# Fifteen block products instead of eighteen: the first layers from expert 1 on by a Hopcroft-Kerr scheme, in a three-stage kernel on one Trainium2 core

## The reference

```python
def _attn_ref(r, k, v, w, u):                      # (2, 8, 768, 48)
    for t in range(S):
        cur = einsum('bhd,bhe->bhde', u * k_t, v_t)
        y[:, :, t] = einsum('bhd,bhde->bhe', r_t, state + cur)
        state = w * state + einsum('bhd,bhe->bhde', k_t, v_t)

def _moe_ref(x, domain_probs, w1, w2):             # x (1536, 384), w1 (4, 384, 1024)
    p = domain_probs / (domain_probs.sum(-1, keepdims=True) + 1e-09)
    for e in range(E):
        out += p[:, e:e + 1] * (np.maximum(x @ w1[e], 0.0) @ w2[e])

def _moe2_ref(x, w_in, w_out):                     # w_in (384, 2048), w_out (2048, 384)
    h = x @ w_in
    return (h * (1.0 / (1.0 + np.exp(-1.702 * h)))) @ w_out
```

## Time and profile before

| what | value |
|---|---|
| median of 3 runs | 642.78 us (642.29 to 642.92) |
| span of the profiled execution, first to last instruction | 640.5 us |
| PE busy | 635.2 us, 3880 matmuls |
| VectorE busy | 222.4 us |
| ScalarE busy | 203.4 us |
| GpSimd busy | 170.0 us |
| granted TensorE clock, mean | 1.000 |

### The profile page before, as it was taken

How to read it: one execution, slowest core, us unless ns; L and a number is a source line. 1 busy time by engine, 2 the same in 40 slices (tenths; PEclk the granted TensorE clock), 3 DMA queues, 4 the chain that set the end, 5 groups by cost and what they waited for, 6 DMA issues and landing times.

```text
span 640.5 us, 9440 instructions
## 1 busy us (share of the span) xinstructions
PE 635.2 (99%) x3880; PEld 529.3 (83%) x3880; DVE 222.4 (35%) x369; ACT 203.4 (32%) x421; POOL 170.0 (27%) x168
## 2 busy tenths in 40 slices
PE   8999999999999999999999999999999999999998
PEld 6999888888888888888888888888888888888886
DVE  8987642212121212121212121213533333333332
ACT  4744432332222212222211223223643333333223
POOL 5664300342242303242402245422750000000000
PEclk9999999999999999999999999999999999999999
DMA  8765521006000501000310000220000010001001
GB/s 331 278 217 189 202 115 51 4 1 247 1 0 1 196 2 49 2 0 1 151 47 1 0 1 0 98 101 1 2 0 1 3 47 1 0 2 50 1 0 50
DMA packets 8722, 39.08 MB, mean 61 GB/s; under 512 B 1504, under 2 KB 1632, under 8 KB 7392
## 3 DMA queue, kind: packets, MB, share of 16 engines
q1 hardware_dynamic: 8672, 38.40, 15.9%
HBM read 36.01 MB, written 2.38 MB: 60 GB/s over the span
## 4 chain that ended last, share of the span: by engine, by line
PE 98%; DVE 1%; DMA 0%; issue 0%; ACT 0%; DVEq 0%
PE bank L1097 46%; PE bank L1123 31%; PE bank L1139 15%; PE bank L1171 2%; PE bank L1215 1%; PE bank L1218 1%; PE bank L1205 1%; PE bank L1190 1%; PE bank L1208 0%; DMA wu_sb<-wu_rows 0%; DVE w_pow L800 0%; DVE q_k_mid L816 0%; PE bank L1223 0%; DVE q_tab_k L807 0%; DVE acc L951 0%
## 5 line engine op out<-in xcount | busy, mean ns | idle before, releaser
L1097 PE MATMUL bank<-x_hi,w_hi 128*128 128x512 f32 (+1 forms) x456 | 172.5, 378 | 0.0
L1097 PE MATMUL bank<-x_lo,w_hi 128*128 128x512 f32 (+1 forms) x456 | 172.4, 378 | 0.0
L1097 PE MATMUL bank<-x_hi,w_lo 128*128 128x512 f32 (+1 forms) x456 | 172.3, 378 | 0.0
L876 DVE SCALAR_TENSOR_TENSOR h_lo<-bank,h_hi 128x512 fp32r<-128x512 f32 (+1 forms) x104 | 67.5, 649 | 257.3 <-ACT h_hi L700 257.3
L700 ACT ACTIVATE h_hi<-bank 128x512 fp32r<-128x512 f32 (+1 forms) x104 | 58.7, 564 | 286.6 <-PE bank L1097 286.6
L622 POOL TENSOR_TENSOR w_lo<-staging,w_hi 128x384 fp32r<-128x384 f32 x80 | 82.2, 1039 | 173.4 <-ACT w_hi L670 173.4
L1123 PE MATMUL bank<-h_hi,w_hi 128*128 128x512 f32 (+1 forms) x312 | 117.7, 377 | 0.1
L1123 PE MATMUL bank<-h_hi,w_lo 128*128 128x512 f32 (+1 forms) x312 | 116.3, 373 | 0.0
L1123 PE MATMUL bank<-h_lo,w_hi 128*128 128x512 f32 (+1 forms) x312 | 116.3, 373 | 0.0
L1097 PEld LDWEIGHTS bank<-x_hi,w_hi 128*128 128x128 f32 x456 | 85.8, 188 | 15.9
L1097 PEld LDWEIGHTS bank<-x_hi,w_lo 128*128 128x128 f32 x456 | 85.8, 188 | 15.8
(11 more groups left out here) (86 smaller groups left out, 433.4 us busy)
## 6 DMA issues: line engine op xcount, KB each, us to landing
staging<-weights SPq DMA_DIRECT2D x10, 1536.0 KB, 8.7
rkv_in<-rkv_n SPq DMA_DIRECT2D x10, 640.0 KB, 5.5
rk_in<-rk_t SPq DMA_DIRECT2D x12, 512.0 KB, 5.2
staging<-weights SPq DMA_DIRECT2D x4, 768.0 KB, 8.9
p_bc<-p_normalised SPq DMA_DIRECT2D x4, 768.0 KB, 4.2
out<-p_bc SPq DMA_DIRECT2D x9, 256.0 KB, 2.1
rkv_in<-rkv_n SPq DMA_DIRECT2D x2, 448.0 KB, 5.7
u_bc<-u_rows SPq DMA_DIRECT2D x1, 192.0 KB, 11.7
```

The costliest lines, as they stand in the source:

```text
L876: dve.scalar_tensor_tensor(h_lo[:, slot, 0:size], hid, 0.0, h_hi[:, slot, 0:size].bitcast(F32), ALU.max, ALU.subtract).then_inc(sem["hlo"], 1)
L1097: last = pe.matmul(bank[:, HID[j % 2], 0:tokens.stop - tokens.start], w[:, k, :], xs[c][:, k, tokens], start=(n == 0), stop=(n == 3 * KT - 1))
```

## The change

Experts 1 to 3 and the second feed-forward block are worked in **pairs** of hidden tiles: a pair q is two hidden tiles by all three token blocks, four pairs to a stage, 20 in all (0 to 11 the experts, 12 to 19 the second block). The first layer of a pair is a product of a 2 x 3 matrix of weight blocks by a 3 x 3 matrix of x blocks (128 features by 512 tokens). Written plainly that is 18 block products of three matmuls. The new kernel uses 15: each multiplies a sum of weight blocks (12 sums, made anew per pair, `weight_sums`) or a weight block itself by a sum of x blocks (8 summed blocks, made once for the experts by `form(0, ...)` and once for the second feed-forward block by `form(1, ...)`, rounded and split by `sum_high` and `sums_low`) or an x block.

A product writes one of three banks (5, 6, 7; the third column of `PRODUCT`). Where `begins` is False it adds to what is there. Behind each product the bank is read once: by ScalarE, which copies it, with a sign, to one of eight result buffers t (`take`, 6 per pair), or by VectorE, which adds or subtracts it (`join`, 9 per pair). When the last product of a result is in, ScalarE rounds it (`high`) and VectorE, in the second block GpSimd, makes the low part (`low`). In the second block sigmoid (`silu`, ScalarE) and `gate` (VectorE) come before.

The second layer of a pair is nine **groups** of 6 matmuls (token block n, output tile k; two hidden tiles by three passes). For n = 0 they stay in PSUM over the four pairs of a stage, for n = 1 and 2 they leave after every pair (`leave` on VectorE, the exit; for the experts then `gather` on GpSimd). In the list of the program five products of pair q + 1 follow one group of pair q, then come two groups more and the next, and so on. Pair 12 (`PLAIN`), the first of the second feed-forward block, has its first layer done plainly, in 6 products of 9 matmuls, since its input is only then finished; it comes between the groups of pair 11 (which all leave), and pair 13 is mixed into it in another pattern. Weights are loaded per pair (384 KB for each layer) in place of per stage. The sums of blocks for the second block stand in VectorE's queue behind the third gate of pair 12, their low parts in GpSimd's at the same place of the list.

```diff
-STEPS1 = MOE_BLOCKS * FT
-STEPS = STEPS1 + BLOCKS * F2 // P
+STEPS = len(SPANS) * FT
...
+ONE, LONG, SHORT = 7, 5, 6
+PRODUCT = (
+    (0, (1, 1), ONE, True, "copy", 1, 1),
+    (1, 13, LONG, True, "copy", 4, -1),
+    (2, (0, 0), SHORT, True, "copy", 0, 1),
+    (3, (2, 1), LONG, False, "add", 1, -1),
+    (12, 8, SHORT, False, "add", 1, -1),
+    (4, (1, 0), ONE, True, "add", 0, 1),
+    (13, 14, LONG, False, "add", 0, 1),
+    (5, 3, SHORT, False, "copy", 2, 1),
+    (6, 9, LONG, False, "copy", 3, 1),
+    (7, (2, 2), ONE, True, "copy", 5, -1),
+    (8, (0, 2), SHORT, False, "add", 5, 1),
+    (9, 1, ONE, False, "add", 3, -1),
+    (14, 10, LONG, False, "add", 5, 1),
+    (10, 4, SHORT, False, "add", 4, -1),
+    (11, (1, 2), LONG, False, "add", 2, 1),
+)
+SUM_HOME = {13: 0, 8: 1, 14: 2, 3: 3, 9: 4, 1: 5, 10: (0, 1), 4: (2, 0)}
+SUM_ORDER = (13, 8, 14, 3, 9, 1, 10, 4)
...
+def pairs():
+    order = [("product", 0, i) for i in range(PRODUCTS)]
+    begin = {0: 0}
+    def mix(q, lead):
+        begin[q + 1] = len(order)
+        left = iter(range(PRODUCTS))
+        for n, takes in enumerate(lead):
+            if n:
+                order.append(("group", q, *divmod(n - 1, KT)))
+            order.extend(("product", q + 1, next(left)) for _ in range(takes))
+    for q in range(PLAIN - 1):
+        mix(q, (0, 5, 0, 0, 5, 0, 0, 5, 0, 0))
+    q = PLAIN - 1
+    begin[PLAIN] = len(order)
+    order += [("group", q, n, k) for n in range(2) for k in range(KT)] + [("plain", PLAIN, i) for i in range(2)]
+    order += [("group", q, 2, k) for k in range(KT)] + [("plain", PLAIN, i) for i in range(2, 6)]
+    mix(PLAIN, (0, 0, 0, 0, 0, 2, 1, 2, 2, 8))
+    for q in range(PLAIN + 1, ALL_PAIRS - 1):
+        mix(q, (0, 5, 0, 0, 5, 0, 0, 5, 0, 0))
+    begin[ALL_PAIRS] = len(order)
+    order += [("group", ALL_PAIRS - 1, n, k) for n in range(BLOCKS) for k in range(KT)]
+    after = [[] for _ in range(len(order) + 8)]
+    for at, (what, q, *rest) in enumerate(order):
+        if what == "product" and rest[0] in (LAST_OF[o] for o in DONE):
+            pos = DONE.index(PRODUCT[rest[0]][5])
+        elif what == "plain":
+            pos = rest[0]
+        else:
+            if what == "group" and q == PLAIN - 1:
+                after[at + 2].append(("rest", q, *rest))
+            continue
+        later = iter(range(at + 1, at + 5))
+        if q >= MOE_PAIRS:
+            after[next(later)].append(("silu", q, pos))
+            after[next(later)].append(("gate", q, pos))
+        after[next(later)].append(("high", q, pos))
+        after[next(later)].append(("low", q, pos))
+    for q in range(1, ALL_PAIRS):
+        at = begin[q - 1]
+        if q == PLAIN:
+            after[at + 4].append(("weight", q, 0))
+        else:
+            for i, way in enumerate((0, 1, 2)):
+                after[at + i].append(("sum", q, way))
+            for i, piece in zip((3, 4, 5, 6, 7), range(len(PIECES))):
+                after[at + i].append(("weight", q, piece))
+    for q in range(ALL_PAIRS):
+        after[begin[q] + 9].append(("second", q))
+    out = []
+    for at in range(len(after)):
+        out += order[at:at + 1] + after[at]
+    return out
...
@@ gpsimd @@
+    def sums_low(turn, blocks):
+        for i, op in enumerate(SUM_ORDER):
+            pool.wait_ge(sem["shi"], len(SUM_ORDER) * turn + i + 1)
+            pool.tensor_tensor(sum_home(s_lo, x_lo, op), blocks[FORMED[op][0]], sum_home(s_hi, x_hi, op).bitcast(F32),
+                               ALU.subtract).then_inc(sem["slo"], 1)
...
+    for what, q, *rest in PAIR_LIST:
+        if what == "group" and (q, *rest) in LEAVES and q < MOE_PAIRS:
+            gather(q, *rest)
+        elif what == "weight":
+            weight_low(q, *rest)
+        elif what == "second" and q:
+            second_low(q)
+        elif what == "low" and q >= MOE_PAIRS:
+            tile_low(q, *rest)
+        elif what == "plain" and rest[0] == 5:
+            sums_low(1, blocks1)
...
@@ scalar @@
+    def take(q, i):
+        _, _, at, _, _, o, sign = PRODUCT[i]
+        number = t_number(q, o)
+        act.wait_ge(sem["prod"], PRODS[q] + i + 1)
+        if number >= T_RING:
+            done, value = t_before(number)
+            act.wait_ge(sem[done], value)
+        act.activation(t_of[number % T_RING], bank[:, at, :], ACT.Copy, scale=float(sign)).then_inc(sem["copied"], 1)
...
+    for what, q, *rest in PAIR_LIST:
+        if what == "product" and rest[0] in COPIED:
+            take(q, *rest)
+        elif what == "group" and q == PLAIN - 1:
+            plain_high(*rest)
+        elif what == "weight":
+            weight_high(q, *rest)
+        elif what == "second" and q:
+            second_high(q)
+        elif what == "silu":
+            tile_silu(q, *rest)
+        elif what == "high":
+            tile_high(q, *rest)
+            if q == PLAIN and rest[0] == 5:
+                for i in range(len(SUM_ORDER)):
+                    sum_high(1, blocks1, i)
...
@@ vector @@
+    def join(q, i):
+        _, _, at, _, _, o, sign = PRODUCT[i]
+        t = t_of[t_number(q, o) % T_RING]
+        before = [x for x in ADDED if x < i and PRODUCT[x][5] == o]
+        dve.wait_ge(sem["prod"], PRODS[q] + i + 1)
+        if before:
+            dve.wait_ge(sem["added"], JOINED[q] + ADDED.index(before[-1]) + 1)
+        else:
+            dve.wait_ge(sem["copied"], TAKEN[q] + COPY_OF.index(o) + 1)
+        if sign > 0:
+            dve.tensor_tensor(t, bank[:, at, :], t, ALU.add).then_inc(sem["added"], 1)
+        else:
+            dve.scalar_tensor_tensor(t, bank[:, at, :], -1.0, t, ALU.mult, ALU.add).then_inc(sem["added"], 1)
...
+        elif j == JOIN + 6:
+            weight_sums(0, 0)
+            weight_sums(0, 1)
+            weight_sums(0, 2)
+    dve.wait_ge(sem["slo"], len(SUM_ORDER))
+    evacuate(len(SPANS) - 1)
+    for what, q, *rest in PAIR_LIST:
+        if what == "product" and rest[0] in ADDED:
+            join(q, *rest)
+        elif what == "group":
+            if (q, *rest) in LEAVES:
+                leave(q, *rest)
+        elif what == "sum":
+            weight_sums(q, *rest)
+        elif what == "gate":
+            tile_gate(q, *rest)
+        elif what == "low" and q < MOE_PAIRS:
+            tile_low(q, *rest)
+        elif what == "rest":
+            plain_low(*rest)
+        elif what == "plain" and rest[0] == 5:
+            form(1, blocks1, 0, FORMINGS)
...
@@ tensor @@
+    def product(q, i):
+        weight, rows, at, begins, _, _, _ = PRODUCT[i]
+        piece = next(n for n, (first, last) in enumerate(PIECES) if first <= weight < last)
+        pe.wait_ge(sem["alo"], PARTS_W[q] + piece + 1)
+        if q in (0, PLAIN + 1) and type(rows) is int:
+            pe.wait_ge(sem["slo"], len(SUM_ORDER) * (q > 0) + SUM_ORDER.index(rows) + 1)
+        if q == PLAIN + 1 and begins and i < 3:
+            pe.wait_ge(sem["gate"], 6)
+        earlier = [x for x in range(i) if PRODUCT[x][2] == at]
+        if earlier:
+            x, before = earlier[-1], q
+        elif q and q != PLAIN + 1:
+            x, before = max(x for x in range(PRODUCTS) if PRODUCT[x][2] == at), q - 1
+        else:
+            x = None
+        if x in COPIED:
+            pe.wait_ge(sem["copied"], TAKEN[before] + COPIED.index(x) + 1)
+        elif x in ADDED:
+            pe.wait_ge(sem["added"], JOINED[before] + ADDED.index(x) + 1)
+        for n, (a, c) in enumerate(PASSES):
+            last = pe.matmul(bank[:, at, :], a_parts[a][:, q % 2, weight * P:(weight + 1) * P], rows_of(ss[c], xs[c], rows),
+                             start=(begins and n == 0), stop=(n == 2), skip_group_check=True)
+        last.then_inc(sem["prod"], 1)
...
+    def group(q, n, k):
+        begins, ends = (kept_first(q), kept_last(q)) if n == 0 else (True, True)
+        if n == 0:
+            at = KEPT[k]
+            if q == 0:
+                pe.wait_ge(sem["ev1"], KT * len(SPANS))
+            elif begins:
+                pe.wait_ge(sem["evac"], LEAVES[q - 1, 0, k] + 1)
+        else:
+            at = shared_bank(q, n, k)
+            number = shared_number(q, n, k)
+            if number >= len(SHARED):
+                pe.wait_ge(sem["evac"], LEAVES[shared_at(number - len(SHARED))] + 1)
+        pe.wait_ge(sem["vlo"], q + 1)
+        for f in range(2):
+            number = 6 * q + place_of(q, f, n)
+            done, value = low_tile(number)
+            pe.wait_ge(sem[done], value)
+            for i, (a, c) in enumerate(PASSES):
+                last = pe.matmul(bank[:, at, :], v_parts[a][q % 2][:, f * DM + k * P:f * DM + (k + 1) * P], tiles[c][number % H_RING],
+                                 start=(begins and f == 0 and i == 0), stop=(ends and f == 1 and i == 2))
+        last.then_inc(sem["grp"], 1)
```

639 lines of the change are left out of this document (423 added, 216 removed).

## The result

The changed kernel takes **677.7 us** (median of 4 runs, 677.1 to 678.8) beside 642.5 us of the kernel before (642.2 to 642.9): a ratio of 1.0551, 95% interval 1.0536 to 1.0566. It is slower, as forecast, but by 35 us where 20 were forecast, 0.7 us above the upper end of the range.

A forecast was written before the change was run, and what follows sets the result against it. PE was taken as the bound, matmul count times spacing. 171 fewer matmuls saved 38.8 us; waits of 13.2 + 9.6 + 5.0 + 25.9 + 3.3 + 1.6 + 0.1 gave +19.9, forecast 662 us, range 648 to 677.

The forecast's parts named there:

- hand-over chain: Product waiting for its bank's reader: 0.45 + 0.43 + 0.60 or 0.69 + 0.22 = 1.70 (ScalarE) or 1.79 us (VectorE); PE comes after 1.36.
- first seam: Pair 0, after expert 0: product 6 waits for product 3's join behind 12 weight sums; with smaller waits +5.0 us (3 to 6).
- long stop: Pair 12's fourth group waits 18.3 us for low tiles behind eight low block sums on GpSimd, themselves behind VectorE's 13 sums.
- Rival 1: Bank hand-overs are hidden, PE's next product comes after 1.36 us all the same; some 22 us of holds vanish: 640; chance 0.08.
- rival 2: The second seam is shorter, at its low end of 16 us: 652; chance 0.13.
- Rival 4: Short holds take the clock to its lower level for half of each of 19 pairs: about 870; chance 0.02.
- second seam: Around pairs 11 and 12, where the second block's input and summed blocks must be finished: +25.9 us (16 to 30).
- +1.6 (0 to 4): Behind the long stop, eight matmuls run at half rate: 8 x (0.43 - 0.23) = +1.6 us.
- Pairs 1 to 11: 11 x 1.2: Hand-over holds of 0.34, 0.43 and 0.43 us at products 3, 8 and 14 in each pair: +13.2 us.
- rival 3: GpSimd's longer weight pieces delay the fourth exit's gather, so product 12's join comes 1 us late in 11 pairs: 673; chance 0.13.
- steps before pair 0: From step 24 at 112.92, eight steps of 4.08 us put product 0 of pair 0 near 147.6; no added wait.
- full lock: VectorE operations with two SBUF inputs wait out whole GpSimd instructions, short weight sums up to 1.3 us: sum 5 us higher.

The follow-up runs named there:

- e1_spread: The changed kernel with a pair's products spread three, two, three, two, three, two in a row, a second-layer group between, in place of fives: 666.6 us.
- e4_first_sums: The changed kernel with the weight sums and weight roundings of pair 1 six places later in the order: 675.3 us.
- e2_low_moved: The changed kernel with GpSimd's eight low parts of the second block's summed blocks behind pair 12's sixth low tile, not ahead of its third: 671.0 us.
- e3_form_moved: The changed kernel with VectorE's 13 block sums of the second block behind gate 3 of pair 12, not ahead of it: 677.8 us.
- e7_low_later: e1_spread with VectorE's low part of a pair's first hidden tile, in experts 1 to 3, behind the joins of products 5 and 6: 659.2 us.
- e5_weights_late: e2_low_moved with the weight sums, roundings and low parts of pair 13 eight places later, behind the exits and gathers of pair 11: 670.1 us.
- e6_all: The changed kernel with products spread, weights of pairs 1 and 13 later, low block sums behind the sixth tile, block sums behind gate 3: 652.0 us.
- e8_joined: e6_all with the low part behind joins 5 and 6, second-seam weight sums and GpSimd work reordered, one product of pair 13 moved later: 647.2 us.
- e10_turn: e8_joined with the five weight pieces three places apart, in place of in a row, in pairs where an expert ends: 644.2 us.
- e12_split: The kernel with all earlier reorderings together (640.4 us), the last four of 13 block sums moved behind the fourth and fifth plain groups' exits: 640.2 us.

## Why the prediction was right and wrong

**Right.** The sign, and why: 171 matmuls fewer were worth 38.8 us, and waits took it back. The hand-over chain of 1.79 us stands in the trace link by link (1.80 for product 14), with holds at products 3, 8 and 14 in the pairs from 1 on: 0.33, 0.55 and 0.43, in sum 1.3 for 1.2 forecast (more at product 8 in pairs 4 and 8, and at product 3 from pair 14 on). The first seam's wait for the join behind weight sums (2.9) and the cause of the long stop are as written; e1_spread bears out the hand-over, e4_first_sums the first seam, e2_low_moved and e3_form_moved the long stop. Rival 1 (hidden hand-overs) fell with every hold, rival 2 with a seam of 26.9 us for 25.9. Rival 4 fell too: over fifty short holds left the clock at its upper level. The rule named beside rival 4 (the Trainium skill, TensorE: Matmul & The Clock Gate, "A second HAM failure mode: psum-queue depth-cycling"), by which short idle times of PE between groups of matmuls, as it cycles through PSUM banks, make the clock swing between its levels, did not come to bear in this kernel: 1.00 granted through pairs 1 to 11.

**Right by luck: the sum of the second seam.** Its 26.9 us, for 25.9 forecast, are other waits than those forecast. Forecast were 3.7 ahead of the first plain product, 3.9 ahead of the fifth and 18.3 for the long stop. Measured were 4.3 ahead of the sixth group of pair 11 and 1.8 ahead of its last group (both for exits), 6.3 ahead of the fifth plain product and 14.2 for the long stop. Errors of up to 4.1 us cancelled.

**Wrong: the time.** The mechanism and the direction held, the size of the sum did not: 677.7 us for a forecast of 662 and a range of 648 to 677. All high ends together gave 678 in the prediction itself. The terms that were mis-sized follow, the largest first.

**Wrong: "+1.6 (0 to 4)" for the cold clock.** The step that failed was to count only the longest stop. The clock also fell behind waits of 2.9, 4.3 and 6.3 us, so it cost 7.75 us, 6.2 more than forecast. Behind the long stop itself eight matmuls ran at the lower clock, as forecast: the price of a matmul there and the number for one occasion were right, the number of occasions was wrong (14, 8, 9 and 8 matmuls).

**Wrong: "Pairs 1 to 11: 11 x 1.2".** It measured 18.6. A usual pair takes 1.42 longer than its matmuls, so 11 of them 15.6 us; and in pairs 4 and 8 product 8 waits 2.0 in place of 0.55, because an exit waits for a gather behind weight pieces on GpSimd. In pair 4, VectorE then GpSimd:

```profile
248.78 0.69 DVE L1401 TENSOR_TENSOR part<-bank,p_bc 128x512 f32<-128x512 f32 x1 [1.28 <-POOL acc L837]
```
```profile
244.25 2.70 POOL L825 TENSOR_TENSOR a_lo<-staging,a_hi 128x768 fp32r<-128x768 f32 x3 [2.19 <-ACT a_hi L990]
246.90 1.75 POOL L837 TENSOR_TENSOR acc<-acc,part 128x512 f32<-128x512 f32 x1
```

That is rival 3's mechanism, forecast for all pairs as a rival or for none; it is in two of them, 3.0 us. The step that failed was "each fits": it was worked out for a pair with six exits, not for one with nine.

**Wrong: steps before pair 0 at nothing.** In the steps before the first pair PE waits once, 1.7 us, for a low part behind four block sums which took 1.46 to 1.78 us each beside GpSimd. The prediction named a price of 0.7 for such meetings and applied it to the pairs, not here.

**One cause behind several.** VectorE and GpSimd hinder each other in SBUF often by more than the 0.7 assumed: an operation of 0.28 us takes 1.35, one of 0.68 up to 2.3 and once 4.6. e7_low_later shows what one such meeting per pair in front of a join costs (7.3 us over the kernel); for the steps before pair 0 and for the seams it is read from the traces alone, and no run prices it. In the prediction the full lock stood as a sentence beside the sum with 5 us for it. Of the 15 us missed, 6.2 are the clock, 5.4 the pairs 1 to 11, 1.65 the steps, 1.2 the last pairs, and the rest is 1 us or less each.

What stays open is what decides whether a wait of 2 to 3 us lowers the clock; it moves single executions of these kernels by about 2 us.

## What to carry to other kernels

Matmuls taken from a bound PE pay only if the work that replaces them keeps off PE's chains; read for every bank how long its reader holds it and put that much other PE work between. Where VectorE operations with both inputs in SBUF meet GpSimd's, their times should be summed, not laid side by side, and such an operation should not stand directly ahead of one that PE waits for. When a stop is removed, look at the sum over the stretch: here three repairs in the same 60 us each removed their own wait and moved it on.

## What the runs showed of the hardware

- Beside GpSimd, VectorE's operations with both inputs in SBUF took up to 1.9 us for 128 columns (0.28 alone; 1.35 in a row of them beside a row of GpSimd's) and mostly up to 2.4 for 512 (0.68 alone). Joins and exits, which read PSUM, kept 0.69 in every trace. GpSimd's were drawn out too: up to 1.75 for a tile's low part of 1.28 in the changed kernel.
- An operation can be held for longer than one of the other engine's: in e5_weights_late a VectorE sum of 0.68 us took 4.61 beside three of GpSimd's in a row, and in e6_all a weight piece of 1.85 us on GpSimd took 4.50 (from 457.76) beside six block sums of VectorE in a row.
- In the changed kernel the granted clock fell to its lower level with waits of 2.9, 4.3, 6.3 and 14.2 us and stayed up through waits of 0.3 to 2.1. A wait of 2.0 to 2.1 us inside the first group of pair 13 stands in ten traces: the clock fell at it or within 1.5 us behind it in seven (e1 to e6 and e8_joined) and not in three (the changed kernel, e7_low_later and e10_turn). In e12_split it stayed up through one of 2.9.
